# The tail group's reciprocal joined to the next iteration's first group, and its transposes set behind the next second product

## The reference

```python
scores = scale * np.matmul(q, k.transpose(0, 1, 3, 2))
mask = (rel >= 0) & (rel < window)
scores = np.where(mask, scores + bias[None], -1000000000.0)
scores = scores - np.max(scores, axis=-1, keepdims=True)
attn = np.exp(scores)
attn = attn / (np.sum(attn, axis=-1, keepdims=True) + 1e-09)
out = np.matmul(attn, v)
...
logits = x @ w_gate          
for e in range(E):
    h = np.maximum(x @ w1[e], 0.0)
    out += P[:, e:e + 1] * (h @ w2[e])
...
h = x @ w_in
return np.maximum(0.01 * h, h) @ w_out
```

## Time and profile before

| | us |
|---|---|
| median of 3 runs | 2050.15 |
| lowest, highest | 2049.0, 2050.66 |
| the profiled execution | 2049.61 |
| its span, first to last instruction | 2047.8 |
| mean granted TensorE clock | 0.999 of full |

### The profile page before, as it was taken

The page is one execution under the profiler, slowest core; times in us unless marked ns, Lnnn a source line. Parts: engine busy times, 40 slices in busy tenths (PEclk is TensorE's granted clock), DMA queues, the critical chain, the costliest instruction groups (busy, mean ns, idle before and its releaser), DMA issues.

```text
span 2047.8 us, 36400 instructions
## 1 busy us (share of the span) xinstructions
PE 2032.2 (99%) x12475; PEld 1815.3 (89%) x12475; DVE 1183.9 (58%) x2708; ACT 643.1 (31%) x1776; POOL 1167.4 (57%) x1451
## 2 busy tenths in 40 slices
PE   8999999999999999999999999999999999999999
PEld 6788999899999899999999999999999989998998
DVE  8876766555555555564555554554554565667666
ACT  8972222222222222233222222222222244334332
POOL 3425556555566565576555566655555575667551
PEclk9999999999999999999999999999999999999999
DMA  5311111111111111111111111111111111111211
GB/s 178 119 66 42 42 42 41 51 41 51 41 41 41 51 41 51 41 37 47 42 52 41 51 41 41 41 51 41 51 41 41 41 41 52 42 52 56 73 42 47
DMA packets 31311, 104.86 MB, mean 51 GB/s; under 512 B 3968, under 2 KB 4480, under 8 KB 31232
## 3 DMA queue, kind: packets, MB, share of 16 engines
q1 hardware_dynamic: 31232, 103.84, 15.1%
HBM read 99.11 MB, written 4.72 MB: 51 GB/s over the span
## 4 chain that ended last, share of the span: by engine, by line
PE 95%; DVE 2%; POOL 1%; ACT 1%; issue 1%; DMA 0%; SPq 0%; ACTq 0%; DVEq 0%; POOLq 0%
PE bank L1227 16%; PE bank L1228 16%; PE bank L1229 16%; PE bank L1205 14%; PE bank L1208 14%; PE bank L1207 14%; PE bank L1146 1%; PE bank L1124 1%; PE bank L1116 1%; PE bank L1159 1%; ACT sc L541 1%; DVE sc L792 1%; POOL up_lo L369 0%; DVE sc L776 0%; PE bank L1243 0%
## 5 line engine op out<-in xcount | busy, mean ns | idle before, releaser
L876 DVE SCALAR_TENSOR_TENSOR acc<-bank,gate,acc 128x512 f32<-128x512 f32 x495 | 371.6, 751 | 573.8 <-PE bank L1229 573.8
L1205 PE MATMUL bank<-x_hi,up_hi 128*128 128x256 f32 (+1 forms) x2240 | 663.3, 296 | 2.0 <-POOL up_lo L369 1.9
L1208 PE MATMUL bank<-x_hi,up_lo 128*128 128x256 f32 (+1 forms) x2240 | 662.9, 296 | 0.0
L1207 PE MATMUL bank<-x_lo,up_hi 128*128 128x256 f32 (+1 forms) x2240 | 662.3, 296 | 0.0
L1228 PE MATMUL bank<-down_lo,hs_hi 128*128 128x512 f32 x1440 | 568.0, 394 | 0.0
L1227 PE MATMUL bank<-down_hi,hs_hi 128*128 128x512 f32 x1440 | 567.5, 394 | 0.4 <-DVE hs_lo L990 0.4
L1229 PE MATMUL bank<-down_hi,hs_lo 128*128 128x512 f32 x1440 | 560.3, 389 | 0.0
L1205 PEld LDWEIGHTS bank<-x_hi,up_hi 128*128 128x128 f32 x2240 | 423.9, 189 | 30.0 <-POOL up_lo L369 2.7
L1207 PEld LDWEIGHTS bank<-x_lo,up_hi 128*128 128x128 f32 x2240 | 423.9, 189 | 23.6
L1208 PEld LDWEIGHTS bank<-x_hi,up_lo 128*128 128x128 f32 x2240 | 423.8, 189 | 0.0
L369 POOL TENSOR_TENSOR up_lo<-stage_up,up_hi 128x256 fp32r<-128x256 f32 x546 | 384.7, 742 | 6.3
(11 more groups left out here) (118 smaller groups left out, 1823.1 us busy)
## 6 DMA issues: line engine op xcount, KB each, us to landing
stage_up<-w_up SPq DMA_DIRECT2D x80, 512.0 KB, 3.4
stage_down<-w_down SPq DMA_DIRECT2D x80, 512.0 KB, 3.4
qk<-qk SPq DMA_DIRECT2D x15, 608.0 KB, 3.8
v_nat<-v SPq DMA_DIRECT2D x16, 320.0 KB, 2.9
result<-acc SPq DMA_DIRECT2D x16, 256.0 KB, 2.6
result<-acc SPq DMA_DIRECT2D x4, 128.0 KB, 3.0
qk<-qk SPq DMA_DIRECT2D x2, 128.0 KB, 2.1
qk<-qk SPq DMA_DIRECT2D x1, 192.0 KB, 2.5
```

The source lines that it names most:

```text
L876: last = d.scalar_tensor_tensor(out=to, in0=y[:, :], scalar=share(g, tile, e), in1=to, op0=ALU.mult, op1=ALU.add)
L1205: m.matmul(to[:, 0:n], up_hi[s][:, w], x_hi[u][:, x], start=first and c == 0, stop=False, skip_group_check=True)
L1207: m.matmul(to[:, 0:n], up_hi[s][:, w], x_lo[u][:, x], start=False, stop=False, skip_group_check=True)
L1208: last = m.matmul(to[:, 0:n], up_lo[s][:, w], x_hi[u][:, x], start=False, stop=c == 1, skip_group_check=True)
```

## The change

The tail of iteration i and group 0 of iteration i+1 now share one addition of EPS and one reciprocal, on 128 rows and six columns. For this the columns of `esum`, `esum_eps` and `einv` are laid out anew (`STAT_AT`), so that the two columns of the tail stand beside the four of the other buffer's group 0; `esum` is filled with 1.0 once at the start, since the tail has only 64 rows. Both scalings follow, the tail's first, in `normalise_two`. It stands where group 0 was normalised before, so the tail is normalised later, behind the bias of group 1 of i+1. On TensorE the tail's transposes move from the end of step i into step i+1, behind its values of group 1, and directly ahead of the transposes of group 0; the wait inside the values of group 0 goes.

```diff
+    STAT_AT = ((2, 6, 10), (12, 16, 0))
...
+            d.memset(esum[:, :], 1.0)
...
+            def inverses(rows, st0, ends, n):
+
+                st = slice(st0, ends)
+                d.tensor_scalar_add(esum_eps[0:rows, st], esum[0:rows, st], EPS).then_inc(eps_added, 1)
+                dve.wait_ge(eps_added, n + 1)
+                d.reciprocal(einv[0:rows, st], esum_eps[0:rows, st]).then_inc(inv_done, 1)
+                dve.wait_ge(inv_done, n + 1)
...
+            def normalise_two(i, s, n):
+
+                dve.wait_ge(exp_done, GROUPS * (i + 1) + 1)
+                inverses(P, STAT_AT[s][2], STAT_AT[s][2] + 6, n)
+                scale(2, s)
+                scale(0, 1 - s)
...
                 bias_scores(i, 2, s, pair)
-                normalise(i, 1, s)
+                normalise(i, 1, s, 2 * i + 1)
                 if last:
                     sums(0, 2)
-                if not last:
+                    normalise(i, 2, s, 2 * i + 2)
+                else:
                     bias_scores(i + 1, 0, 1 - s, after)
-                normalise(i, 2, s)
-                if not last:
                     bias_scores(i + 1, 1, 1 - s, after)
-                    normalise(i + 1, 0, 1 - s)
+                    normalise_two(i, s, 2 * i + 2)
...
-                for n, (hd, t, kt, nk, _, b, to) in enumerate(todo):
-                    if n == len(todo) - 1 and g == 0:
-
-                        pe.wait_ge(normed, GROUPS * i + 3)
+                for hd, t, kt, nk, _, b, to in todo:
...
                 if not first:
                     values(i - 1, 1, 1 - s)
+                    pe.wait_ge(normed, GROUPS * i)
+                    transpose_p(2, 1 - s)
...
-                transpose_p(2, s)
...
             step(ITERS - 1, 1, last=True)
+            pe.wait_ge(normed, GROUPS * ITERS)
+            transpose_p(2, 1)
             values(ITERS - 1, 1, 1)
             values(ITERS - 1, 2, 1)
```

More of the change, by code:

```diff
@@ L164, in segments @@
         def segments(g, s):
-            sc0, st0 = s * SLOTS * 512, s * STATS
+            sc0, st0 = s * SLOTS * 512, STAT_AT[s][g]
             if g == GROUPS - 1:
                 nk = P + TAIL
-                return [(hd, QT, (QT - 1) * P, nk, 0, sc0 + 2 * g * 512 + hd * nk, st0 + 4 * g + hd) for hd in range(2)]
+                return [(hd, QT, (QT - 1) * P, nk, 0, sc0 + 2 * g * 512 + hd * nk, st0 + hd) for hd in range(2)]
             got = []
@@ L176, in segments @@
                     slot = 2 * g + hd
-                    got.append((hd, t, max(t - 1, 0) * P, nk, c, sc0 + slot * 512 + c, st0 + 2 * slot + n))
+                    got.append((hd, t, max(t - 1, 0) * P, nk, c, sc0 + slot * 512 + c, st0 + 2 * hd + n))
             return got
@@ L780, in bias_scores, with scale @@
                 last.then_inc(biased, 1)
-            def normalise(i, g, s):
-                rows = rows_of(g)
[L784 to L789, removed]
+            def inverses(rows, st0, ends, n):
[4 more added lines that the diff above has]
+                dve.wait_ge(inv_done, n + 1)
+            def scale(g, s):
+                rows = rows_of(g)
                 for _, _, _, nk, _, c, st in segments(g, s):
@@ L793, in normalise @@
                 last.then_inc(normed, 1)
+            def normalise(i, g, s, n):
+                dve.wait_ge(exp_done, GROUPS * i + g + 1)
+                inverses(rows_of(g), STAT_AT[s][g], STAT_AT[s][g] + len(segments(g, s)), n)
+                scale(g, s)
+            def normalise_two(i, s, n):
[3 more added lines that the diff above has]
+                scale(0, 1 - s)
             def sums(first, ends):
@@ L824, in _ @@
             bias_scores(0, 1, 0, 0)
-            normalise(0, 0, 0)
+            normalise(0, 0, 0, 0)
             dve.wait_ge(bias_sel, 2)
```

## The result

| | before | changed |
|---|---|---|
| median, us | 2050.12 | 2053.65 |
| lowest to highest | 2049.0 to 2051.53 | 2052.53 to 2055.81 |
| runs | 20 | 20 |
| profiled execution (span) | 2049.61 (2047.8) | 2053.91 (2052.1) |

The changed kernel takes 3.53 us longer; the ratio of the times is 1.0017, with a 95% interval of 1.0011 to 1.0023. That is a real loss, and it lies inside the 0.2% that the prediction called no change. The times of both kernels fall in two groups some 1.2 us apart, nine executions in the lower and eleven in the upper one, and the changed kernel is some 3.6 us later in either.

A forecast was written before the change was run, and what follows sets the result against it. TensorE was taken to bound the kernel, attention's time passing on one to one. Terms 1.6 - 0.2 + 1.4 + 0.1 + 0.4 - 0.25, say +3.0 on 2049.61, plus 0.54 for the median, gave 2053.1 us; range 2049.8 to 2055.8.

The forecast's parts named there:

- What bounds: Whole kernel: TensorE is busy 99% of the span, so what attention takes is passed on one to one.
- The loop: First four attention steps: the tail's scaling enters the wait loop through VectorE, 7.27 to 7.74 us a step; +1.6 us.
- Catching up, -0.2: Attention step 4, which took 8.03 us before, should now take TensorE's own 7.85; -0.2 us.
- TensorE's sum stays 7.86.: Attention steps with logits: moving the tail's transposes on TensorE leaves its total per step unchanged, so costs nothing.
- The meetings: Steps 6 to 14: GpSimd pieces begin inside group 0's scaling and stretch it beyond the slack; +1.4, +0.1 and +0.4 us.
- The reciprocal pair, nothing: VectorE, fifteen times: removing one sum and reciprocal of 0.38 us saves 5.7 us of work but only idle time.
- The last step, -0.25: Last attention step: group 0's values no longer wait for the tail's scaling, group 1's transposes come 0.17 later; -0.25 us.
- (a): Rival, attention scalings: GpSimd loses the port each time, so only the loop costs; +1.2, 2051.4 us, chance 0.18.
- (c): Rival, ten steps: GpSimd's pair also meets group 1's scaling, +0.4 each; in all +7, 2057.1 us, chance 0.12.
- (d): Rival, nine GpSimd meetings: full blocking costs 0.27 more each; in all +5.4, 2055.6 us, chance 0.08.
- (e): TensorE's half-speed clock dip from 104 us, some 1.7 us: absent gives 2051.4, a second 2054.8; no chance of its own.

The follow-up runs named there:

- e3: Changed kernel with GpSimd's pieces that the tail's scores released now released by the next iteration's group 0 scores; median 2052.56 us, ratio 1.0012 to the kernel before.
- e2: Changed kernel with the tail's and group 0's sum and reciprocal computed as two pairs again, at the joint place; median 2056.25 us, ratio 1.003 to the kernel before.
- e4: Changed kernel with group 1's values ahead of the tail's scores on TensorE; median 2053.43 us, ratio 1.0012 to the kernel before.
- e5: Kernel before with GpSimd's pieces that the tail's scores released now released by the next iteration's group 0 scores; median 2052.99 us, ratio 1.0013 to the kernel before.
- e6: Changed kernel with group 0's scaling ahead of the tail's on VectorE and its transposes ahead on TensorE; median 2057.7 us, ratio 1.0039 to the kernel before.
- e7: Kernel before run and profiled once more, no edit; median 2050.53 us, ratio 1.0002.
- e8: Changed kernel run and profiled once more, no edit; median 2053.97 us, ratio 1.002 to the kernel before.
- e9: Text leaves open which: changed kernel with the tail's scaling left out (2050.84 us), or with e3's and e4's edits together (2050.81 us); e10 is the other.
- e10: Text leaves open which: changed kernel with e3's and e4's edits together (2050.81 us), or with the tail's scaling left out (2050.84 us); e9 is the other.
- e1: Kernel before with only the tail's transposes moved on TensorE, behind the tail's scores and group 1's values; median 2050.69 us, ratio 0.9999 to the kernel before.

## Why the prediction was right, and where it was not

The forecast was 2053.1 us and the median is 2053.65. Part of that closeness is luck: two errors in opposite directions partly cancel. By parts, 1.6 - 0.2 = 1.4 was worked out for the first steps, 1.9 for the rest of the loop and -0.25 for the end; measured were 0.40 + 0.88 = 1.28, 2.66 and -0.42 (T1's starts, 0.13 of the 2.66 being step 15).

- **What bounds.** Confirmed. What attention lost is what the span lost.
- **The loop.** Confirmed in mechanism and size. 7.74 was worked out, 7.72 measured where nothing stretches (step 4, and steps 2 to 4 of e3); leaving out the tail's scaling takes it back to 7.44. By T0's starts the first four steps took 42.62 - 9.90 = 32.72, of which some 0.8 is the half rate of the first pieces (last section): 31.9 for the 31.97 predicted.
- **Catching up, -0.2.** Wrong. T0 of iteration 4 starts at 42.62 and that of 5 at 50.62 (a row of T2 and T0 together begins at 50.24, and T2 takes 0.38 of it): 8.00 us, where it was 8.03. The step assumed TensorE's own 7.85, and that sum is 8.00 now.
- **"TensorE's sum stays 7.86."** It became 8.00. This is the step that failed, and the reason of the one before. It added the pieces of one order and took them for those of another. T2 and S2 cost 0.76 us as neighbours and 0.91 apart. Ten steps bound by TensorE (5 to 10 and 12 to 15) carry 0.13 to 0.15 each, 1.4 us that no term held. A row that could have warned stood in the earlier trace rows: T2 is there with three of its four transposes, as its last one runs beside S2's first matmul.
- **The meetings.** Confirmed in place and stretch: the scaling is stretched in 6, 7, 10, 11, 13 and 14, and by 0.57, 0.49 and 0.36 us where 0.55, 0.45 and 0.33 were worked out. The waits of T0 came in 6, 7 and 11 (0.29, 0.15 and 0.47 us); the 0.2 to 0.5 us named for 10, 13 and 14 did not, T0 was 0.09 late. Their cost in time was mis-sized: 1.23 us with step 11 (e3), where 1.4 + 0.1 + 0.4 = 1.9 was predicted. The longer sum of TensorE had widened the slack at T0 from 0.12 to some 0.27 us, so 0.36 came of the 0.43 in step 6, 0.22 of the 0.31 in step 7, and some 0.09 of the 0.21 in 10, 13 and 14, where T0 hardly waits. In step 11, which has the slack of neither, the meeting cost 0.39 for the 0.33 worked out. In step 8 group 0's scaling was not held: VectorE was first, and the cast that began in the last of its instructions took 1.26 us instead of 1.04. It held the next sum instead (0.43 us for 0.15), which nothing waited for.

  From step 5 on, then: 1.9 predicted for the meetings and 1.23 measured, nothing predicted for the order and 1.4 measured; the two measured, with 0.03 that the loop cost in step 11, make up the 2.66 of the table.
- **The reciprocal pair, nothing.** Confirmed. The 5.7 us of VectorE's work went to its idle time; the changed kernel's VectorE stands idle for 1.30 us ahead of S1's scores in step 7, where it was 0.58. e2 shows the pair worth 0.4 us a step in the loop that the change makes.
- **The last step, -0.25.** V0's twelve went from 1.30 to 0.88 us, as predicted, -0.42 by T1's starts; T1 itself is 0.13 later, so -0.29.

Of the rivals, (a) is out, since T0's waits and the stretches are there (its sum was too high as well: without stretches the first four steps would cost 4 x 7.74 - 30.37 = 0.6 and not 1.6, so (a) stood for 2050.4 us); (c) did not come about in the changed kernel, whose margin held, but it is real: e4, e5 and e6 each ran into it. For (d), full blocking, the scaling instruction that the cast of 57.36 held, VectorE in order of time:

```profile
57.54 0.85 DVE L796 TENSOR_SCALAR sc<-sc,einv 128x128 f32<-128x128 f32 x1
```

The cast ended at 58.31 and this instruction at 58.39. With its whole 0.27 us behind the cast it would have ended at 58.58, 0.19 later, so (d) is out, and it would have cost less than the 0.27 a meeting that it was priced at. Where the Trainium skill (SBUF — State Buffer, section Who interferes with whom) has the second fully blocked, the stretches here are the piece's length without the meeting less some 0.25 us. On (e), the drop did not vanish but moved, below.

The Trainium skill (TensorEngine Tiling (Array Packing), section Key Properties) says that a change of tiling mode drains TensorE. T2 and S2 have 64 rows, their neighbours V1, T0 and the logits 128. If the rows alone made the mode, the old order would change it twice there and the new one four times; no trace shows the mode, and by the columns V1 (128*64) differs from its 128-row neighbours as well. The traces would fit such a price, 0.17 us for two changes of rows fewer in e4. They don't show whether it is the drain or the lost overlap of T2 with S2; both go with the neighbourhood, and no run took them apart.

What stays open is that, and why the clock falls where it does; the first would take a kernel in which 64-row pieces are neighbours but cannot overlap.

## What to carry to other kernels

A sum over an engine's pieces holds for their order alone: when a change moves a piece, look at the edges it leaves and gets, above all where small matmuls of the same shape class stood together. Sharing a small operation is worth its length only where it is waited for, and here the sharing itself moved other work into that place. And when a piece of GpSimd's meets a scaling, look for where it lands when either is moved: three of the five edits that moved one of them (e4, e5, e6) loaded another scaling.

## What the runs showed of the hardware

The granted clock fell to 0.50 (1.2 of 2.4 GHz) for some three microseconds in each of these four profiles, but not at the same place: at 104 us in the first one of the kernel before, from 139 us in that of the changed kernel, and from 11 us in e7 and e8, the same two kernels. It belongs to an execution, not to a kernel. At 104 us TensorE had been without a gap since 95.88 and at 139 since 136.30; at 11 us it had just begun, behind more than 2 us idle. Stretches of one microsecond, of the changed kernel and of the kernel before (e7):

```profile
140.00:141.00 1.00, 1.00 (x14) 0.90 (x10) 0.77 (x2) 0.82 (x2) 0.00 (x0) 0.50 0.00 0
```

```profile
12.00:13.00 1.00, 0.81 (x4) 0.82 (x5) 1.00 (x9) 0.62 (x4) 0.94 (x2) 0.50 0.46 188
```

TensorE can also be slow where the profile shows the clock at full. Its first pieces in the changed kernel, and the same in e7:

```profile
9.90 1.54 PE L1139 MATMUL bank<-ident,sc 128*128 128x128 f32 x6 [2.33 <-DVE sc L796]
11.37 1.65 PE L1131 MATMUL bank<-qk 64*128 64x128 f32 x8
```

```profile
9.97 0.88 PE L1124 MATMUL bank<-ident,sc 128*128 128x128 f32 x6 [2.34 <-DVE sc L792]
10.78 1.19 PE L1116 MATMUL bank<-qk 64*128 64x128 f32 x8
```

1.54 for 0.88 us behind an idle time of 2.33 us, with the column at 1.00. The same 1.54 us at 1.00 stand in e3, e4, e6, e9 and e10; in e8, the changed kernel again, it is 0.87. So it comes and goes with the execution. Whether the kernel before has it too is open: e1 and e5, with its order on VectorE, start slowly as well (1.18 and 1.40 us), but with the column falling to 0.50. Nor do the runs show whether at 1.00 the column missed such a drop or the cause is another. In the changed kernel's first profile it moved everything behind it by 0.8 us, a quarter of the effect measured here, which is why the steps are compared from step 2 on.
